# Fused attention, rational MLP and soft MoE on one core: combine in packed f32 tiles, first turn of g at its step's end, fourth w_in block in one piece, single x buffers, ten early pieces

## The chip, the cores and the metric

The kernel runs on one core of a Trainium2 chip. The metric is the device time of one execution in microseconds (us); lower is better. TensorE (PE, with its weight loads PEld), VectorE (DVE) and ScalarE (ACT) run their own instruction streams and meet at semaphores; SyncE (SP) issues nearly all DMAs.

## What is computed

```python
# attention: B=4, H=8, S=768, D=64; chunks of 32 queries, 16 keys to the left, 8 to the right, 8 memory keys
a = softmax(scale * q_c @ k_full.T); out[:, :, c] = a @ v_full
x = out.transpose(0, 2, 1, 3).reshape(3072, 512)
# rational MLP: w_in 512 x 2048, w_out 2048 x 512
h = x @ w_in
g = (a0 + a1*h + a2*h*h + a3*h*h*h) / (1 + |b0|*|h| + |b1|*h*h + 1e-6)
x = g @ w_out
# soft MoE: 8 experts, 4 slots each, w1 8 x 512 x 1024, w2 8 x 1024 x 512
logits = x @ phi
slot_input = softmax(logits, axis=0).T @ x
slot_out[e] = relu(slot_input[e] @ w1[e]) @ w2[e]
y = softmax(logits, axis=1) @ slot_out
```

## The kernel before

**Tokens.** 24 tiles of 128 tokens (4 batches of 6) go through a software pipeline. One step of each engine works on tile n (the hidden layer), the attention of tile n+1 (`nxt`), the transposes of g and the logits of n-1 (`prev`), the running column softmax of n-2 (`prev2`), and on TensorE the scores of n+2. g @ w_out is never formed per token: `Wp` = w_out @ phi is made once, and the slots accumulate g, which meets w_out at the end.

**Hidden layer.** `hidden` (lines 397 to 413) makes block f (512 columns) of h out of 12 matmuls of 512 columns, with x and w_in each split in a high and a low part (f32r). The blocks alternate between two PSUM banks `hb`. On ACT `hidden_reads` (710) copies hs, |h| and h squared out of the bank, and `inverse` and `inverse2` (721, 725) take Ln and Exp of the denominator; on DVE `cubic` (925) makes the numerator and the denominator q, and `activation` (940) makes g.

**Order within a TensorE step (476 to 548), written out by hand.** hidden 0; g_transposes 0 of prev; hidden 1; g_transposes 1, add_quadrants, p_transposes; hidden 2; attend (L386) of nxt; g_transposes 2 of prev; d_transpose of prev2; the first half of hidden 3; x_transposes of nxt; g_transposes 3; the second half of hidden 3; slots of prev2 (L456); logits of prev (L433); scores of n+2 (L362). `g_transposes` (four transposes, L339) all use the bank `gb`, so each waits until ACT has copied the one before (`gT_copy`, 729). `slots` waits for `dk_sb`, which `d_copy` (958) on DVE sets.

**DVE's order in a step (977 to 1020).** activation 3 of prev, softmax_max of nxt (with a memset for the first and the last tile of a batch, 897 to 902), cubic 0, activation 0, running_max, cubic 1, o_norm of nxt (908, it waits for attend), cubic 2, d_copy of prev2, x_low of nxt (919), activation 1, cubic 3, activation 2, accumulate. **ACT's order (767 to 828):** inverse 3 of prev, part_copy, hidden_reads 0, gT_copy 0, softmax_exp, inverse 0, hidden_reads 1, gT_copy 1, pT_copy (697), dispatch_exp, hidden_reads 2, gT_copy 2, inverse 1, x_high (703), gT_copy 3, hidden_reads 3, inverse 2. x_hi and x_lo have two buffers each.

**Expert weights.** w1 and w2 (32 MB) are 64 pieces of 512 KB ("quarters"), four to a stage, stages 0 to 7 for w1 and 8 to 15 for w2. Seven go to SBUF of their own and are loaded in steps 2 to 5 (285 to 290). The others (297 to 321) go to places that come free only with the last tile: three of the attention (waits on sc_psum, o_psum, xT_psum), sixteen of w_in (each four wait for one hidden block of the last tile, 307), then those of x, g, the temporaries and w_out, then places of used stages. SP issues all of it in order, and the stores of the result behind it (323 to 330).

**End.** The experts run as col-packed matmuls (32 slots wide, L599 and L637). `combine_turns` (613) transposes the softmax over slots, split in a high and a low part, with 48 matmuls of 64 x 128. `slot_rows` (641) replicates the experts' output for half the columns; ACT copies its upper 64 partitions and DVE makes the high and low parts of the other 64 in two steps (1113 to 1116). `combine` (647) then makes 24 f32r matmuls of 256 columns over all 128 partitions (L661), two to a pair of tiles; DVE and ACT copy pairs out in turn (1117, 880), and SP stores two to four pairs at a time. combine(0) runs between stages 13 and 14, combine(1) behind stage 15.

Of the kernel before, what the change touches and what calls it, by code (L numbers as in the profile page):

```python
# [5 lines left out]
def build(nc, qT_d, kw_d, vw_d, w_in, w_out, w_outT, cst_d, w1, w2, out):  # L6
# [23 lines left out]
    with ExitStack() as ctx:  # L30
# [27 lines left out]
        ab = sb("ab", [P, 2, 512])  # L58
        h2 = sb("h2", [P, 2, 512])
        tt = sb("tt", [P, 2, 512])  # L60
        qq = sb("qq", [P, 2, 512])
        early = sb("early", [P, 7168])
# [16 lines left out]
        xn = sc  # L79
        w_raw = [x.rearrange("p (k n) -> p k n", n=512)  # L80
# [5 lines left out]
        c_hl = gT[:, 4:16, :].rearrange("p a (t h s) -> p (a t) h s", h=2, s=NS)  # L86
# [4 lines left out]
        s_hi = g[:, 1, 512:1024]  # L91
# [14 lines left out]
        EARLY, ATT, WF, LATE, LEFT_G, TMP = 7, 3, 16, 2, 2, 5  # L106
# [9 lines left out]
        spots += [in_wout + QB * i for i in range(4)]  # L116
# [3 lines left out]
        def place(stage, c):  # L120
# [5 lines left out]
                   nc.alloc_sbuf_tensor_at("o_b", [P, 4, 2 * HC], f32, offset=in_tmp + 2 * QB),  # L126
# [8 lines left out]
        cT4 = nc.alloc_sbuf_tensor_at("cT4", [P, N, P], f32r, offset=in_wout + 16 * QUARTER)  # L135
        s4 = nc.alloc_sbuf_tensor_at("s4", [P, DM], f32r, offset=in_wout + 16 * QUARTER + 4 * N * P)
# [9 lines left out]
        o_bank = [[at[:, 0, :], at[:, 1, :], gb[:, :]], [at[:, 2, :], sl[:, :], at[:, 0, :], at[:, 1, :], gb[:, :]]]  # L146
# [74 lines left out]
        s4_act = sem("s4_act")  # L221
        s4_dve = sem("s4_dve")
# [14 lines left out]
        def g_bank(n, f):  # L237

            return at[:, f, :] if isinstance(n, int) and n == N - 1 and f < FC - 1 else gb
# [9 lines left out]
        def _(sp):  # L249
# [47 lines left out]
            for i in range(EARLY, 60):  # L297
# [36 lines left out]
        def _(pe):  # L334
# [62 lines left out]
            def hidden(b, t, f, kds=range(KD)):  # L397
# [9 lines left out]
                for kd in kds:  # L407
                    xs = slice(kd * P, kd * P + P)
                    mm(o, x_hi[:, p, xs], w_hi[:, f, kd, :], start=kd == 0, stop=False)  # L409
                    mm(o, x_hi[:, p, xs], w_lo[:, f, kd, :], start=False, stop=False)  # L410
                    i = mm(o, x_lo[:, p, xs], w_hi[:, f, kd, :], start=False, stop=kd == KD - 1)  # L411
# [3 lines left out]
            def g_transposes(b, t, f):  # L415
                n = b * T + t
                pe.wait_ge(g_done, FC * n + f + 1)
                last = isinstance(n, int) and n == N - 1 and f < FC - 1
                if not last:
                    need(pe, gT_sb, FC * n + f - (FC - 1 if isinstance(n, int) and n == N - 1 else 0))  # L420
# [55 lines left out]
            def step(b, t):  # L476
# [22 lines left out]
                if prev:  # L499
                    g_transposes(*prev, 0)  # L500
# [46 lines left out]
                if nxt2:  # L547
                    scores(*nxt2)

# [53 lines left out]
            def expert_turns(grp):  # L603
                for half in range(2):
                    pe.wait_ge((relu_dve, relu_act)[half], grp + 1)
                    if grp:
                        pe.wait_ge((cT_act, cT_dve)[half], N // 8)
# [5 lines left out]
            def combine_turns():  # L613
                pe.wait_ge(comb_step, 8)
                for j in range(N // 4):
                    if j < 2:
                        pe.wait_ge((hT_act, hT_dve)[j], 1)
                    else:
                        pe.wait_ge((cT_act, cT_dve)[j % 2], j // 2)
                    for m in range(4):  # L620
                        x = c_hl[:, 4 * j + m, :, :].rearrange("p a b -> p (a b)")
                        for r in (slice(0, 2 * NS), slice(2 * NS, 4 * NS)):
                            i = mm((gb, mb)[j % 2][r, m * P:m * P + P], x, ident[:, :], start=True, stop=True)
                    i.then_inc(cT_psum, 1)
# [22 lines left out]
            def combine(ch):  # L647
                cs = slice(HC * ch, HC * ch + HC)
                pe.wait_ge(s4_act, ch + 1)
                pe.wait_ge(s4_dve, 2 * ch + 2)  # L650
                if ch == 0:
                    pe.wait_ge(hT_act, 2)
                for j in range(PAIRS):
                    q = PAIRS * ch + (j - len(o_bank[ch]) if j >= len(o_bank[ch]) else -1)
                    if q >= 1:
                        pe.wait_ge((o_dve, o_act)[q % 2], q // 2 + 1)
                        pe.wait_ge((o_act, o_dve)[q % 2], (q + 1) // 2)
                    elif q == 0:
                        pe.wait_ge(o_dve, 1)
                    for m in range(2):  # L660
                        i = mm(o_bank[ch][j % len(o_bank[ch])][:, HC * m:HC * m + HC], cT4[:, 2 * j + m, :], s4[:, cs],  # L661
# [516 lines left out]
```

## Time and profile before

| | us |
|---|---|
| median of 3 runs | 527.86 (527.72 to 528.7) |
| profiled execution, its own time | 529.32 |
| its span | 527.4 |
| PE busy | 509.8 (97%) |
| DVE busy | 445.0 (84%) |
| ACT busy | 401.3 (76%) |

The span is what the profile shows of the execution. Busy time is the union of an engine's instructions. Stretches and rows below are in us from the span's start. In a timeline row the second number is the duration; successive instructions of an engine overlap in part, so prices are best read from start to start.

### The profile page before, as it was taken

The numbers are of one execution on the slowest core, as the hardware profiler recorded it, in microseconds if no ns is written. First come the engines' busy times: TensorE is split into PE (matmuls) and PEld (weight loads), VectorE is DVE, ScalarE is ACT, GpSimd is POOL, SyncE is SP. The second block draws the span as 40 slices with busy tenths as digits, with TensorE's granted clock in tenths as the row PEclk, the third lists the DMA queues.
The fourth block names the chain that finished last, engine by engine and source line by source line (L and its number), as shares of the span: only waits on it lengthen the run. The fifth ranks groups of instructions, "written<-read, shape, count | busy, mean of one in ns | idle before, by whom it ended". The sixth has DMA issues, their size and how long they took to land.

```text
span 527.4 us, 15890 instructions
## 1 busy us (share of the span) xinstructions
PE 509.8 (97%) x6610; PEld 387.0 (73%) x6610; DVE 445.0 (84%) x828; ACT 401.3 (76%) x778; POOL 0.2 (0%) x4
## 2 busy tenths in 40 slices
PE   8899999999999999999999999999999999999983
PEld 7667877877787778778777877787787777645543
DVE  5898999999999999999999999999999999642143
ACT  1878989888988898898889888988988898512032
POOL 0000000000000000000000000000000000000000
PEclk9999999999999999999999999999999999999996
DMA  8983275335122311312131322113122227999997
GB/s 346 416 334 119 64 262 180 121 105 181 43 93 70 103 43 62 101 57 87 62 103 43 88 74 78 68 62 102 58 87 61 83 81 289 412 408 409 408 410 298
DMA packets 23400, 85.31 MB, mean 162 GB/s; under 512 B 2593, under 2 KB 2721, under 8 KB 21409
## 3 DMA queue, kind: packets, MB, share of 16 engines
q1 hardware_dynamic: 23184, 84.09, 43.6%
q8 instruction: 53, 0.87, 0.7%
q10 hardware_dynamic: 144, 0.20, 0.1%
q14 instruction: 19, 0.15, 0.1%
HBM read 77.99 MB, written 6.29 MB: 160 GB/s over the span
## 4 chain that ended last, share of the span: by engine, by line
PE 89%; DMA 4%; ACT 2%; SPq 1%; DVE 1%; issue 1%; ACTq 0%
PE hb L409 18%; PE hb L411 17%; PE hb L410 17%; PE gb L339 9%; PE sl L456 4%; PE at L339 4%; PE mb L433 4%; PE at L386 3%; PE at L362 3%; DMA place<-w 2%; DMA g<-w_in 2%; PE at L599 1%; PE hb L599 1%; PE mb L441 1%; PE hb L345 1%; ACT w_hi L835 1%
## 5 line engine op out<-in xcount | busy, mean ns | idle before, releaser
L409 PE MATMUL hb<-w_hi,x_hi 128*128 128x512 f32 x384 | 162.6, 423 | 1.1 <-DVE x_lo L922 1.1
L411 PE MATMUL hb<-w_hi,x_lo 128*128 128x512 f32 x384 | 151.9, 396 | 0.0
L410 PE MATMUL hb<-w_lo,x_hi 128*128 128x512 f32 x384 | 151.3, 394 | 0.0
L716 ACT ACTIVATE hs<-hb 128x512 f32<-128x512 f32 x96 | 57.2, 596 | 48.0 <-PE hb L411 46.8
L411 PEld LDWEIGHTS hb<-w_hi,x_lo 128*128 128x128 f32 x384 | 72.2, 188 | 17.8
L409 PEld LDWEIGHTS hb<-w_hi,x_hi 128*128 128x128 f32 x384 | 72.2, 188 | 15.4 <-issue 1.4
L410 PEld LDWEIGHTS hb<-w_lo,x_hi 128*128 128x128 f32 x384 | 72.5, 189 | 11.9
L931 DVE SCALAR_TENSOR_TENSOR qq<-h,few,ab 128x512 f32<-128x512 f32 x96 | 71.9, 749 | 10.6 <-ACT h L718 10.4
L936 DVE SCALAR_TENSOR_TENSOR tt<-tt,cst,hs 128x512 f32<-128x512 f32 x96 | 72.2, 752 | 3.4
L723 ACT ACTIVATE qq<-qq,few 128x512 f32<-128x512 f32 x96 | 70.2, 732 | 5.8 <-DVE qq L931 4.4
L946 DVE SCALAR_TENSOR_TENSOR g<-tt,cst,qq 128x512 f32<-128x512 f32 x96 | 71.5, 747 | 2.3 <-ACT qq L727 0.2
L717 ACT ACTIVATE ab<-hb,cst 128x512 f32<-128x512 f32 x96 | 65.8, 686 | 0.0
L934 DVE TENSOR_TENSOR tt<-tt,hs 128x512 f32<-128x512 f32 x96 | 65.8, 686 | 0.0
L727 ACT ACTIVATE qq<-qq 128x512 f32<-128x512 f32 x96 | 60.7, 632 | 3.1
L339 PE MATMUL gb<-cst,g 128*128 128x128 f32 x380 | 58.5, 277 | 1.2 <-DVE g L1095 0.8
L718 ACT ACTIVATE h<-hb 128x512 f32<-128x512 f32 x96 | 57.9, 604 | 0.0
L733 ACT ACTIVATE gT<-gb 128x512 f32<-128x512 f32 x93 | 56.6, 609 | 0.7 <-PE gb L339 0.7
L929 DVE TENSOR_SCALAR tt<-hs,cst 128x512 f32<-128x512 f32 x96 | 52.1, 543 | 2.9 <-ACT hs L716 0.4
L339 PEld LDWEIGHTS gb<-cst,g 128*128 128x128 f32 x380 | 44.3, 140 | 13.4 <-DVE g L1095 2.6
L339 PE MATMUL at<-cst,sc 128*128 128x128 f32 x192 | 29.7, 277 | 1.5 <-ACT sc L694 1.1
L433 PEld LDWEIGHTS mb<-gT,Wp 128*32 128x32 f32 x736 | 20.9, 110 | 13.5 <-issue 13.5
L339 PEld LDWEIGHTS at<-cst,sc 128*128 128x128 f32 x192 | 23.7, 149 | 6.3 <-ACT sc L694 1.8
(154 smaller groups left out, 548.1 us busy)
## 6 DMA issues: line engine op xcount, KB each, us to landing
place<-w SPq DMA_DIRECT2D x60, 512.0 KB, 10.3
v_in<-v_windows SPq DMA_DIRECT2D x24, 520.0 KB, 3.8
kw<-k_windows SPq DMA_DIRECT2D x24, 512.0 KB, 4.6
qT<-q_t SPq DMA_DIRECT2D x24, 256.0 KB, 2.7
wout<-w_out_t SPq DMA_DIRECT2D x4, 1024.0 KB, 14.7
wout<-w_out SPq DMA_DIRECT2D x4, 1024.0 KB, 6.7
g<-w_in SPq DMA_DIRECT2D x3, 1024.0 KB, 10.5
out_dram<-o_c SPq DMA_DIRECT2D x6, 512.0 KB, 4.9
```

Of the source, the lines that this page charges most:

```text
L339: return mm(dst, src, ident[0:rows, 0:rows], start=True, stop=True, is_transpose=True)
L409: mm(o, x_hi[:, p, xs], w_hi[:, f, kd, :], start=kd == 0, stop=False)
L410: mm(o, x_hi[:, p, xs], w_lo[:, f, kd, :], start=False, stop=False)
L411: i = mm(o, x_lo[:, p, xs], w_hi[:, f, kd, :], start=False, stop=kd == KD - 1)
L717: A(ab[:, e, :], hb[:, e, :], ACT.Abs, scale=bc[:, 0:1])
L718: A(h2[:, e, :], hb[:, e, :], ACT.Square).then_inc(h_read, 1)
L723: A(qq[:, e, :], qq[:, e, :], ACT.Ln, bias=cq[:, 0:1]).then_inc(ln_done, 1)
L727: A(qq[:, e, :], qq[:, e, :], ACT.Exp, scale=-1.0).then_inc(r_done, 1)
L931: V.scalar_tensor_tensor(out=qq[:, e, :], in0=h2[:, e, :], scalar=bm[:, 1:2], in1=ab[:, e, :], op0=ALU.mult, op1=ALU.add).then_inc(q_done, 1)
L934: V.tensor_tensor(tt[:, e, :], tt[:, e, :], hs[:, e, :], ALU.mult).then_inc(poly_step, 1)
L936: V.scalar_tensor_tensor(out=tt[:, e, :], in0=tt[:, e, :], scalar=pc[:, 1:2], in1=hs[:, e, :], op0=ALU.add, op1=ALU.mult).then_inc(poly_st ...
L946: V.scalar_tensor_tensor(out=g[:, t % 3, 512 * f:512 * f + 512], in0=tt[:, e, :], scalar=pc[:, 0:1], in1=qq[:, e, :], op0=ALU.add, op1=ALU ...
```

## The change

It lays out memory anew (pT shares sc, one x_hi and one x_lo, one ab, no qq: q is written over h2), which makes room for ten early pieces in place of seven. On TensorE g_transposes 0 moves to the end of its own step, g_transposes 3 goes right behind 2, with 2 in the bank at[:, 2], attend moves behind d_transpose, hidden 3 is one piece, and x_transposes comes behind it. The combine is made of plain f32 matmuls over 32 rows, four to a round in different banks, with six transposes in place of the 48 matmuls.

```diff
-        pT = sb("pT", [P, HP * P])
-        x_hi = sb("x_hi", [P, 2, KD * P], f32r)
-        x_lo = sb("x_lo", [P, 2, KD * P], f32r)
+        x_hi = sb("x_hi", [P, KD * P], f32r)
+        x_lo = sb("x_lo", [P, KD * P], f32r)
-        early = sb("early", [P, 7168])
+        early = sb("early", [P, 10240])
+        pT = sc[:, :, :, :].rearrange("p a b c -> p (a b c)")
-        EARLY, ATT, WF, LATE, LEFT_G, TMP = 7, 3, 16, 2, 2, 5
+        EARLY, ATT, WF, LATE, LEFT_G, TMP = 10, 3, 16, 1, 2, 3
-        spots += [in_wout + QB * i for i in range(4)]
+        spots += [in_wout + QB * i for i in (0, 1, 2, 3, 6, 7)]
-        o_bank = [[at[:, 0, :], at[:, 1, :], gb[:, :]], [at[:, 2, :], sl[:, :], at[:, 0, :], at[:, 1, :], gb[:, :]]]
+        o_bank = [at[:, 0, :], at[:, 1, :], gb[:, :], at[:, 2, :], sl[:, :]]
...
         def g_bank(n, f):
+            if n == N - 1:
+                return at[:, f, :] if f < FC - 1 else gb
+            return at[:, 2, :] if f == 2 else gb
...
-                if n < 6:
+                if n < 7:
                     for i in range(2 * (n - 2), min(2 * n - 2, EARLY)):
...
-                elif i == RING - 4 or i == RING - 2:
-                    sp.wait_ge(si_psum, (i - RING + 4) // 2 + 1)
+                elif RING - 6 <= i < RING and (RING - i) % 2 == 0:
+                    sp.wait_ge(si_psum, (1, 2, 4)[(i - RING + 6) // 2])
...
@@ x_transposes
                 pe.wait_ge(soft, SOFT * n + SOFT)
+                need(pe, gT_sb, FC * (n - 2) + FC - 1)
...
@@ g_transposes
+                if n < N - 1 and f != 2:
+                    need(pe, gT_sb, FC * n + min(f, 2))
+                elif n < N - 1:
+                    need(pe, pT_sb, min(n + 3, N))
+                elif f == FC - 1:
+                    pe.wait_ge(gT_sb, FC * n)
...
@@ TensorE step
-                if prev:
-                    g_transposes(*prev, 0)
                 if here:
                     hidden(*here, 1)
...
                 if here:
                     hidden(*here, 2)
-                if nxt:
-                    attend(*nxt)
                 if prev:
                     g_transposes(*prev, 2)
+                if prev and not drain:
+                    g_transposes(*prev, 3)
...
                 if prev2:
                     d_transpose(*prev2)
                     spin_drain(b, t, 1)
-                if here:
-                    hidden(*here, 3, range(0, KD // 2))
+                if nxt:
+                    attend(*nxt)
+                if here:
+                    hidden(*here, 3)
...
                 if nxt:
                     x_transposes(*nxt)
-                if prev and not drain:
-                    g_transposes(*prev, 3)
-                if here:
-                    hidden(*here, 3, range(KD // 2, KD))
...
                 if nxt2:
                     scores(*nxt2)
+                if here:
+                    g_transposes(*here, 0)
...
@@ combine_turns
-                pe.wait_ge(comb_step, 8)
-                for j in range(N // 4):
...
+                pe.wait_ge(comb_step, 7)
+                pe.wait_ge(hT_act, 1)
+                for m in range(4):
+                    i = transpose(gb[:, m * P:m * P + P], c_all[:, m * P:m * P + P])
+                i.then_inc(cT_psum, 1)
+                pe.wait_ge(hT_dve, 1)
+                for m in range(2):
+                    i = transpose(mb[:, m * P:m * P + P], c_all[:, (4 + m) * P:(5 + m) * P])
+                i.then_inc(cT_psum, 1)
...
@@ combine
+                nb = len(o_bank)
+                for a in range(PAIRS // 4):
                     for m in range(2):
-                        i = mm(o_bank[ch][j % len(o_bank[ch])][:, HC * m:HC * m + HC], cT4[:, 2 * j + m, :], s4[:, cs],
-                               start=True, stop=True)
-                    i.then_inc(o_psums, 1)
+                        for r in range(4):
+                            j = 4 * a + r
+                            q = PAIRS * ch + (j - nb if j >= nb else -1)
+                            if m == 0 and q >= 0:
+                                pe.wait_ge((o_dve, o_act)[q % 2], q // 2 + 1)
+                            if m == 0 and q >= 1:
+                                pe.wait_ge((o_act, o_dve)[q % 2], (q + 1) // 2)
+                            rows = slice(NS * r, NS * r + NS)
+                            i = mm(o_bank[j % nb][:, HC * m:HC * m + HC], cT[rows, 2 * a + m, :], s_rows[rows, cs],
+                                   start=True, stop=True)
+                            if m == 1:
+                                i.then_inc(o_psums, 1)
...
@@ ACT
-                need(act, h_psum, FC * (n - 1))
-                A(x_hi[:, p, :], at[:, 2, :], ACT.Copy).then_inc(x_hi_done, 1)
+                need(act, h_psum, FC * n)
+                A(x_hi[:, :], at[:, 2, :], ACT.Copy).then_inc(x_hi_done, 1)
...
@@ hidden_reads
-                need(act, q_done, m - 1)
                 A(hs[:, e, :], hb[:, e, :], ACT.Copy).then_inc(h_copied, 1)
-                A(ab[:, e, :], hb[:, e, :], ACT.Abs, scale=bc[:, 0:1])
+                need(act, q_done, m)
+                A(ab[:, :], hb[:, e, :], ACT.Abs, scale=bc[:, 0:1])
+                need(act, g_done, m - 1)
                 A(h2[:, e, :], hb[:, e, :], ACT.Square).then_inc(h_read, 1)
...
@@ ACT step
+                if prev and not drain and n != 2:
+                    gT_copy(*prev, 0)
                 if here:
                     hidden_reads(*here, 0)
...
                     gT_copy(*prev, 2)
+                    gT_copy(*prev, 3)
                 if here:
                     inverse(FC * n + 1, 1)
                     inverse2(FC * n + 1, 1)
                 if nxt:
                     x_high(*nxt)
-                if prev and not drain:
-                    gT_copy(*prev, 3)
...
@@ ACT, end
-                A(s4[0:64, cs], mb[0:64, cs], ACT.Copy).then_inc(s4_act, 1)
+                A(s_rows[:, cs], mb[:, cs], ACT.Copy).then_inc(s_kept, 1)
...
@@ DVE step
+                if here:
+                    activation(*here, 1)
                 if nxt:
                     x_low(*nxt)
                 if here:
-                    activation(*here, 1)
                     cubic(*here, 3)
...
@@ DVE, end
-                dve.wait_ge(rep_psum, ch + 1)
-                V.tensor_copy(s_hi[64:128, cs].bitcast(f32r), mb[64:128, cs]).then_inc(s4_dve, 1)
-                dve.wait_ge(s4_dve, 2 * ch + 1)
-                V.tensor_tensor(s4[64:128, cs], mb[64:128, cs], s_hi[64:128, cs], ALU.subtract).then_inc(s4_dve, 1)
```

## Rows read from the trace of the kernel before

**Rows 1.** The page: busy time and share of TensorE.

```profile
PE 509.8 (97%) x6610; PEld 387.0 (73%) x6610; DVE 445.0 (84%) x828; ACT 401.3 (76%) x778; POOL 0.2 (0%) x4
```

**Rows 2.** Chain that ended last, 440 to 528: start, duration, what.

```profile
499.60 11.54 DMA place<-w
...
511.18 1.11 PE hb L637 x16
```

**Rows 3.** Windows: length, busy of PE, PEld, DVE, ACT, POOL; PEclk, DMA share, GB/s.

```profile
434.00:436.00 2.00, 2.00 (x16) 1.56 (x9) 1.89 (x3) 1.94 (x5) 0.00 (x0) 1.00 0.00 0
...
437.20:439.00 1.80, 1.80 (x11) 1.52 (x10) 1.66 (x4) 1.77 (x4) 0.00 (x0) 1.00 0.40 105
439.00:470.00 31.00, 29.33 (x258) 19.64 (x260) 22.76 (x47) 18.43 (x40) 0.00 (x0) 1.00 1.02 404
...
516.00:518.00 2.00, 2.00 (x11) 2.00 (x10) 1.68 (x3) 1.37 (x3) 0.00 (x0) 0.50 0.78 301
```

**Rows 4.** Timeline of TensorE, 214 to 252: start, duration, engine, line, operation.

```profile
232.65 1.06 PE L456 MATMUL sl<-g,dk 128*32 128x512 f32 x8
...
235.31 0.50 PE L409 MATMUL hb<-w_hi,x_hi 128*128 128x512 f32 x1
...
238.22 0.60 PE L339 MATMUL gb<-cst,g 128*128 128x128 f32 x4
...
245.63 0.86 PE L386 MATMUL at<-v_in,pT 64*32 64x65 f32 x64
246.42 0.66 PE L339 MATMUL gb<-cst,g 128*128 128x128 f32 x4
246.91 0.27 PE L339 MATMUL mb<-cst,dT 128*128 128x128 f32 x1
...
248.43 0.60 PE L339 MATMUL at<-cst,sc 128*128 128x128 f32 x4
248.87 0.60 PE L339 MATMUL gb<-cst,g 128*128 128x128 f32 x4
...
250.80 1.07 PE L456 MATMUL sl<-g,dk 128*32 128x512 f32 x8
```

**Rows 5.** Timeline of VectorE, 213 to 252.

```profile
216.31 0.75 DVE L931 SCALAR_TENSOR_TENSOR qq<-h,few,ab 128x512 f32<-128x512 f32 x1 [0.41 <-ACT h L718]
...
222.64 0.75 DVE L931 SCALAR_TENSOR_TENSOR qq<-h,few,ab 128x512 f32<-128x512 f32 x1
...
234.46 0.75 DVE L931 SCALAR_TENSOR_TENSOR qq<-h,few,ab 128x512 f32<-128x512 f32 x1 [0.36 <-ACT h L718]
...
240.41 0.75 DVE L931 SCALAR_TENSOR_TENSOR qq<-h,few,ab 128x512 f32<-128x512 f32 x1
...
246.53 0.17 DVE L912 TENSOR_SCALAR mx<-at 128x8 f32<-128x8 f32 x1 [0.22 <-PE at L386]
...
250.08 0.18 DVE L961 COPY dk<-mb 128x32 f32<-128x32 f32 x1
```

**Rows 6.** Timeline of ScalarE, 213 to 252.

```profile
232.76 0.60 ACT L716 ACTIVATE hs<-hb 128x512 f32<-128x512 f32 x1 [0.60 <-PE hb L411]
...
244.49 0.62 ACT L701 ACTIVATE pT<-at 128x512 f32<-128x512 f32 x1
...
249.07 0.60 ACT L707 ACTIVATE x_hi<-at 128x512 fp32r<-128x512 f32 x1
```

**Rows 7.** Timeline of all engines, 460 to 528.

```profile
480.60 1.09 PE L623 MATMUL gb<-cst,gT 128*64 128x128 f32 x16
...
486.34 3.64 PE L599 MATMUL at<-place,g 128*32 128x512 f32 x32
...
503.08 0.73 PE L661 MATMUL at<-s,cT 128*128 128x256 f32 x4
...
514.05 0.43 DVE L1116 TENSOR_TENSOR s<-mb,g 64x256 fp32r<-64x256 f32 x1
...
514.58 0.47 PE L661 MATMUL at<-s,cT 128*128 128x256 f32 x2 [1.03 <-ACT s L879]
```

More of the change, by code:

```diff
@@ L125, in build @@
         o_place = [nc.alloc_sbuf_tensor_at("o_a", [P, 8, 2 * HC], f32, offset=in_wout),
-                   nc.alloc_sbuf_tensor_at("o_b", [P, 4, 2 * HC], f32, offset=in_tmp + 2 * QB),
+                   nc.alloc_sbuf_tensor_at("o_b", [P, 4, 2 * HC], f32, offset=in_tmp + QB),
                    nc.alloc_sbuf_tensor_at("o_c", [P, 12, 2 * HC], f32, offset=in_early)]
@@ L132, in o_out @@
             return o_place[0][:, j, :] if j < 8 else o_place[1][:, j - 8, :]
-        cT4 = nc.alloc_sbuf_tensor_at("cT4", [P, N, P], f32r, offset=in_wout + 16 * QUARTER)
-        s4 = nc.alloc_sbuf_tensor_at("s4", [P, DM], f32r, offset=in_wout + 16 * QUARTER + 4 * N * P)
+        cT = nc.alloc_sbuf_tensor_at("cT", [P, N // 4, P], f32, offset=in_wout + 4 * QB)
+        s_rows = nc.alloc_sbuf_tensor_at("s_rows", [P, DM], f32, offset=in_wout + 4 * QB + N * P)
+        assert N * P + 4 * DM <= 2 * QB
         hb = ps("hb", [P, 2, 512])
@@ L408, in hidden @@
                     xs = slice(kd * P, kd * P + P)
-                    mm(o, x_hi[:, p, xs], w_hi[:, f, kd, :], start=kd == 0, stop=False)
-                    mm(o, x_hi[:, p, xs], w_lo[:, f, kd, :], start=False, stop=False)
-                    i = mm(o, x_lo[:, p, xs], w_hi[:, f, kd, :], start=False, stop=kd == KD - 1)
+                    mm(o, x_hi[:, xs], w_hi[:, f, kd, :], start=kd == 0, stop=False)
+                    mm(o, x_hi[:, xs], w_lo[:, f, kd, :], start=False, stop=False)
+                    i = mm(o, x_lo[:, xs], w_hi[:, f, kd, :], start=False, stop=kd == KD - 1)
                 if kds[-1] == KD - 1:
@@ L606, in expert_turns @@
                     if grp:
-                        pe.wait_ge((cT_act, cT_dve)[half], N // 8)
+                        pe.wait_ge((cT_act, cT_dve)[half], 1)
                     for j in range(4):
@@ L613, in combine_turns @@
             def combine_turns():
-                pe.wait_ge(comb_step, 8)
-                for j in range(N // 4):
[L616 to L624, printed above, removed]
+                pe.wait_ge(comb_step, 7)
[7 more added lines that the diff above has]
+                i.then_inc(cT_psum, 1)
             def expert_out(stage):
@@ L700, in pT_copy @@
                 need(act, o_psum, n)
-                A(pT[:, :], at[:, 2, :], ACT.Copy).then_inc(pT_sb, 1)
+                A(pT, at[:, 2, :], ACT.Copy).then_inc(pT_sb, 1)
             def x_high(b, t):
@@ L793, in step @@
                     part_copy(*prev2)
-                if prev:
+                if n == 2:
+                    gT_copy(*prev, 0)
+                if drain:
                     gT_copy(*prev, 0)
@@ L869, in _ @@
                 if grp:
-                    act.wait_ge(cT_psum, N // 4)
+                    act.wait_ge(cT_psum, 2)
                 A(hT[grp][:, 0:4, :].rearrange("p a b -> p (a b)"), gb[:, :], ACT.Copy).then_inc(hT_act, 1)
-                for j in range(0, N // 4, 2) if grp == 0 else ():
-                    act.wait_ge(cT_psum, j + 1)
+                if grp == 0:
+                    act.wait_ge(cT_psum, 1)
                     act.wait_ge(si_psum, FC)
-                    A(cT4[:, 4 * j:4 * j + 4, :].rearrange("p a b -> p (a b)"), gb[:, :], ACT.Copy).then_inc(cT_act, 1)
+                    A(cT[:, 0:4, :].rearrange("p a b -> p (a b)"), gb[:, :], ACT.Copy).then_inc(cT_act, 1)
             for ch in range(2):
@@ L882, in _ @@
                     act.wait_ge(o_psums, q + 1)
-                    A(o_out(ch, j), o_bank[ch][j % len(o_bank[ch])], ACT.Copy).then_inc(o_act, 1)
+                    A(o_out(ch, j), o_bank[j % len(o_bank)], ACT.Copy).then_inc(o_act, 1)
         @block.vector
@@ L921, in x_low @@
                 dve.wait_ge(x_hi_done, n + 1)
-                V.tensor_tensor(x_lo[:, p, :], at[:, 2, :], x_hi[:, p, :].bitcast(f32), ALU.subtract).then_inc(x_lo_done, 1)
+                V.tensor_tensor(x_lo[:, :], at[:, 2, :], x_hi[:, :].bitcast(f32), ALU.subtract).then_inc(x_lo_done, 1)
             def cubic(b, t, f):
@@ L930, in cubic @@
                 dve.wait_ge(h_read, m + 1)
-                V.scalar_tensor_tensor(out=qq[:, e, :], in0=h2[:, e, :], scalar=bm[:, 1:2], in1=ab[:, e, :],
+                V.scalar_tensor_tensor(out=h2[:, e, :], in0=h2[:, e, :], scalar=bm[:, 1:2], in1=ab[:, :],
                                        op0=ALU.mult, op1=ALU.add).then_inc(q_done, 1)
@@ L1083, in _ @@
             dve.wait_ge(comb_step, 5)
-            V.tensor_tensor(Lall[:, :, :], Lall[:, :, :], cb(cr), ALU.mult).then_inc(comb_step, 1)
-            dve.wait_ge(comb_step, 6)
-            V.tensor_copy(c_hl[:, :, 0, :].bitcast(f32r), Lall[:, :, :]).then_inc(comb_step, 1)
-            dve.wait_ge(comb_step, 7)
-            V.tensor_tensor(c_hl[:, :, 1, :].bitcast(f32r), Lall[:, :, :], c_hl[:, :, 0, :], ALU.subtract
-                            ).then_inc(comb_step, 1)
+            tiles = Lall[:, :, :].rearrange("p (a r m) s -> p m a r s", r=4, m=2)
+            order = c_all.rearrange("p (a m r s) -> p m a r s", m=2, r=4, s=NS)
+            scale = cr.rearrange("p (a r m) -> p m a r", r=4, m=2)
+            for m in range(2):
+                V.tensor_tensor(order[:, m], tiles[:, m], scale[:, m].unsqueeze(3).broadcast_to([P, N // 8, 4, NS]), ALU.mult
+                                ).then_inc(comb_step, 1)
             for grp in range(2):
@@ L1097, in _ @@
                 if grp:
-                    dve.wait_ge(cT_psum, N // 4)
+                    dve.wait_ge(cT_psum, 2)
                 V.tensor_copy(hT[grp][:, 4:8, :].rearrange("p a b -> p (a b)"), mb[:, :]).then_inc(hT_dve, 1)
                 if grp == 0:
+                    dve.wait_ge(cT_psum, 2)
                     dve.wait_ge(si_psum, FC)
-                    for j in range(1, N // 4, 2):
-                        dve.wait_ge(cT_psum, j + 1)
-                        V.tensor_copy(cT4[:, 4 * j:4 * j + 4, :].rearrange("p a b -> p (a b)"), mb[:, :]).then_inc(cT_dve, 1)
+                    V.tensor_copy(cT[:, 4:6, :].rearrange("p a b -> p (a b)"), mb[:, 0:2 * P]).then_inc(cT_dve, 1)
             for ch in range(2):
```

33 lines of the change are left out of this document (10 added, 23 removed).

## The prediction

> **What bounds the kernel now.** First the page's busy line: TensorE is busy 97% of the span [rows 1], so ask where it is the clock of the work and where it only looks so. The chain that ended last, read backwards, answers for the end: its longest link is a load of weights from 499.60 to 511.14, and TensorE's last expert matmuls start at 511.18, when it lands [rows 2]. The windows say when that stream begins: between 434 and 436 the DMA queues move nothing, from 437.2 they start, and from 439 they run at 404 GB/s with a share of 1.02 [rows 3]. That is the end of the last tile's first hidden block, whose w_in places the loads may then take. So the span has two parts: up to that moment (437.0) TensorE's steps set the time, behind it the volume of weights does. A piece of 512 KB (0.524 MB) takes 1.30 us at 404 GB/s; 54 of 64 pieces are behind that point, 70 us of the 74 that pass until 511.14, the rest being the start and the stores that already mix in.
>
> In the first part one step is 18.15 us (slots to slots, 232.65 to 250.80), and I find no wait of TensorE inside it [rows 4]. DVE has waits of its own there [rows 5], so it has a little slack. What matters for a reordering is how close each handover is: d_copy starts at 250.08 and ends at 250.26, slots needs it at 250.80 [rows 4, 5], 0.5 of slack; pT is copied by 245.11, attend starts at 245.63 [rows 4, 6], another 0.5.
>
> **Part 1, three more early pieces.** They are loaded in steps 5 and 6, when the queues are mostly empty; I cost them at nothing. Behind 437 there are 51 pieces in place of 54: 3 x 1.30 = 3.9 us less. The places of w_out now wait for si_psum up to 4, and the queue has three pieces fewer as a cushion; about three pieces (4 us) remain at that wait, so no hole. Bounds: 0 (the earlier stores of the first half mix in ahead of the last load, and TensorE has 5 us more of lead to make them early) and 4.5. I take 3.9, since the stores stand behind all loads in SP's order. The Trainium skill ("DMA: Bandwidth & Descriptors", Queues, rings and completion order) says that descriptors of one queue are consumed in ring order; by that the whole 3.9 stands, and nothing here shows it directly.
>
> **Part 2, order of the step.** The work of TensorE is the same: four hidden blocks, four turns of g at 0.44 (248.43 to 248.87) and so on [rows 4]. Entering or leaving the small tiles costs about 0.1 (scores to hidden: the block takes 2.91 from 235.31 to 238.22, against 2.80 for twelve matmuls in a row); there are as many such changes as before, give or take one. I take 0, bounds -0.2 and +0.1 a step. The Trainium skill ("TensorEngine Tiling (Array Packing)", Key Properties) says that a change of tiling mode drains the engine; charged at that 0.1 for each change of mode, one change more or less in 21 steps would make 2 us, which is inside these bounds.
>
> The handovers are another matter. **d_copy to slots:** DVE does o_norm, cubic 2, d_copy behind attend. From the start of attend it is 0.90 to o_norm and 3.55 on to d_copy (246.53 to 250.08), 0.18 for it and 0.05 to TensorE: 4.68 [rows 4, 5]. Before, slots came 5.17 behind attend. Now attend has gone behind the turns 2 and 3 of g and d_transpose, and between it and slots stand only itself (0.79), hidden 3 (2.91) and x_transposes (0.44): 4.14 [rows 4]. TensorE waits 0.54 in each step. Everything from slots on is then late: slots, logits, scores 2.66 (232.65 to 235.31), less about 0.1 for the exit; turn 0 of g 0.44; hidden 0 to the end of hidden 2 10.32 less 0.44 for that turn (235.31 to 245.63); turns 2 and 3 and d_transpose 0.99 [rows 4]. 4.68 + 2.56 + 0.44 + 9.88 + 0.99 = 18.55, a closed loop from attend to attend. With a restart behind the wait (some 0.05) a step is 18.6, +0.45.
>
> **pT_copy to turn 2 of g:** turn 2 now writes the bank at[:, 2] and waits for pT_copy, 1 us ahead of where attend did. pT's time follows from the end of hidden 3: x_transposes to x_hi 0.64 (248.43 to 249.07), x_hi about 0.5 to the next start, hs to q of block 3 1.70 (232.76 to 234.46), q 3 to q 0 of the next tile 5.95 with DVE at work throughout (234.46 to 240.41), then 4.70 until pT is there (244.49 + 0.62): 13.5 [rows 4 to 6]. From attend this is 3.70 + 13.5 = 17.2, and TensorE comes at 4.68 + 2.56 + 0.44 + 9.88 = 17.56. No wait in an ordinary step. Where the next tile opens or closes a batch the memset makes it 6.33 in place of 5.95 (216.31 to 222.64) [rows 5]: 17.6 with the wake-up, so +0.6 for the step in place of +0.45. So it is a second fence right behind the first.
>
> The 20 loops from step 2 to 22 hold 7 such tiles: 13 x 0.45 + 7 x 0.6 = 10.0. Step 1 has no slots, but the pT loop is 18.4 there: +0.6. Turn 0 of g for tile 22 now stands ahead of the last tile's first block: +0.4. **The stream of weights begins 11.0 late.**
>
> Costed at nothing: the single x buffers (activation 1 and x_low come behind d_copy, two operations of about 0.7, so x_lo is ready 5.9 behind attend; hidden 0 of the next tile starts 4.68 + 2.56 + 0.44 = 7.7 behind it; with the slots wait gone 1.2 of cover is left); single ab and h2 in place of qq (their waits name DVE results at least 2 us old); pT in sc. On ACT gT_copy 0 moves into an idle gap before hidden_reads 0, and x_high ahead of hidden_reads 3 delays that by 0.9, which is in the loop above.
>
> **Part 3, the end.** 48 matmuls from 480.60 to 486.34 [rows 7] become six transposes, 0.7: TensorE is 5.0 earlier, but behind it the last load decides, so this is worth nothing now. Of `slot_rows` DVE's second step goes: ACT's copy of 0.4 alone, -0.5 of the 0.96 behind it. The new combine has 24 plain f32 matmuls of 32 rows; no row shows that form. From the col-packed ones (32 instructions of 512 columns, four abreast, in 3.64 us) one f32 matmul of 256 columns is 2 x 0.228 = 0.455 [rows 7]. Four abreast the 24 take 6 x 0.455 = 2.7; one by one 10.9; now the first combine takes 4.8 and the second 5.2, by the copies. L386, 64 rows by 32 columns, 65 wide, issues 64 in 0.79, less than four abreast would allow (64 x 65 x 2 columns at 2.4 GHz, over 4, is 0.87), so row tiles do overlap; I take four abreast. Then the first pair comes 0.5 later than now, or over 1 us at half clock, which the granted clock of 0.50 at 516 (1.2 of 2.4 GHz, behind waits) makes likely [rows 3]; but behind it the stores, 3.1 MB at 0.4 MB/us, are 8 us and hide most. Sum of the end: -0.5 + 0.6 = 0, bounds -1 and +6 (one by one). The Trainium skill ("TensorEngine Tiling (Array Packing)", Theoretical Speedup) gives up to four times for 32-row tiles; by that the 2.7 stands, which no row here shows.
>
> **Sum.** +11.0 - 3.9 + 0 = +7.1. The profiled execution would go from 529.3 (span 527.4, 1.9 around it) to 536.4. It was 1.5 above the median of the runs shown, 527.9, to which I apply the same difference: 535.0.
>
> **Rivals.** (a) **The handovers hide, the shorter stream wins: faster.** The place is slots: if DVE reaches d_copy 0.5 earlier than I read, or TensorE loses only what its fewer changes of mode give back, the loops cost 0 to 1. Then 0.4 + 0.5 - 3.9 = -3.0: 524.9. It decides where the loss per loop stays under (3.9 - 1.0) / 20 = 0.14 us. Against it: 4.68 against 4.14 is read start to start in one step. Chance 0.10. (b) **Only the pT fence holds**, at 18.39 a step and 18.75 with a memset (slots free): 13 x 0.24 + 7 x 0.6 + 1.0 - 3.9 = +4.4: 532.3. Chance 0.15. (c) **The gain of the stream is lost** to stores or to a half clock behind a longer idle: +11: 538.9. Chance 0.12. (d) **The row tiles don't overlap:** combine(1) 10.9 in place of 5.2, and more at half clock: +6 to +12: 541 to 547. Chance 0.05. (e) Gain and loss cancel within 0.2%: 0.05. My forecast, 533.5 to 537: 0.53.
>
> **How the numbers follow.** 535.0 is the likeliest. The range leaves out about half of (a), and (d): 529.5 to 538.5 (its low end reaches a loss of half the loops; its high end most of (c)). About 0.2% (1.06 us) is what a measurement of this kernel can tell from no change. Slower: 0.53 + 0.15 + 0.12 + 0.05 = 0.85; same 0.05; faster 0.10.
>
> **What would show it.** Steps of 18.6 from slots to slots, and of about 18.75 in seven; a wait of TensorE at L456 for DVE's dk of some 0.5, 20 times; its wait at the turn 2 for ACT's pT only in the tiles with a memset; the first load of the dense stream at 448; the last landing near 518; 70 us between the two. Wrong: steps of 18.15, or the wait at another line; a last load that lands as late behind the first block as before (74); L661's successors one behind another at 0.45.

## The result, and the profile after

The changed kernel takes 535.29 us (median of 4 runs, 534.73 to 536.95) against 527.93 us (4 runs): ratio 1.0138, 95% interval 1.012 to 1.0156, slower by 7.4 us. Its profiled execution was the longest of the four, 536.95 us with a span of 535.2.

The step first. The issue of q for a later tile follows the scores at once, so SP's timeline dates the steps (start, duration, what):

```profile
203.53 0.33 SPq L262 DMA_DIRECT2D qT<-q_t  x1
...
222.27 0.33 SPq L262 DMA_DIRECT2D qT<-q_t  x1
...
241.06 0.33 SPq L262 DMA_DIRECT2D qT<-q_t  x1
...
259.65 0.33 SPq L262 DMA_DIRECT2D qT<-q_t  x1
```

Steps of 18.74, 18.79 (both with a memset) and 18.59 us stand where all steps were 18.15 [rows 4]. The waits name what closes them (engine, line, waited for: total, times, longest):

```profile
PEld sl L460 <- DVE dk L970: 14.6, 23, 0.7
...
PE sl L460 <- DVE dk L970: 9.0, 23, 0.4
```

slots (L456 before, L460 now) waits for DVE's dk 23 times. No such wait stood in the repeated steps before. The matmul itself waits 0.4, its weight load 0.7: the row of PEld counts from the end of the last load, which ran ahead of the matmuls, so the time lost is the matmul's own, 9.0 us in all. TensorE's timeline after, in the step that answers to [rows 4]:

```profile
233.60 0.86 PE L386 MATMUL at<-v_in,sc 64*32 64x65 f32 x64
...
237.30 0.60 PE L339 MATMUL at<-cst,sc 128*128 128x128 f32 x4
...
238.30 1.06 PE L460 MATMUL sl<-g,dk 128*32 128x512 f32 x8 [0.40 <-DVE dk L970]
...
240.96 0.66 PE L339 MATMUL gb<-cst,g 128*128 128x128 f32 x4
...
251.13 0.60 PE L339 MATMUL at<-cst,g 128*128 128x128 f32 x4
...
252.21 0.86 PE L386 MATMUL at<-v_in,sc 64*32 64x65 f32 x64
```

and DVE's, which answers to [rows 5]:

```profile
234.50 0.17 DVE L921 TENSOR_SCALAR mx<-at 128x8 f32<-128x8 f32 x1 [0.95 <-PE at L386]
...
238.06 0.18 DVE L970 COPY dk<-mb 128x32 f32<-128x32 f32 x1
```

attend at 233.60, o_norm 0.90 later, dk copied at 238.24, slots at 238.30: 4.70 behind attend. x_transposes start at 237.30; where nothing waits (attend_pt below, 250.12 to 250.64) slots follow them by 0.52, which would have been 237.82. So 0.48 is lost. Both attends are 18.61 apart.

Now the end. The last tile's first hidden block ends at 448.64 in place of 437.19 (437.0 in the prediction is the start of the turn behind it), 11.4 later. Its last matmul in TensorE's timeline, before and after:

```profile
436.80 0.39 PE L411 MATMUL hb<-w_hi,x_lo 128*128 128x512 f32 x1
...
448.24 0.40 PE L412 MATMUL hb<-w_hi,x_lo 128*128 128x512 f32 x1
```

The chain that ended last, from there on:

```profile
492.48 15.13 DMA place<-w
507.61 0.04 issue
507.65 1.93 PE hb L637 x32
...
516.18 5.84 PE hb L637 x64
```

This is not the end of [rows 2]. The load on the chain is that of stage 13, not the last one; behind it come stage 13, combine(0) (509.58 to 516.18) and stages 14 and 15 in 5.84 us without a wait for weights. 5.84 us for 64 matmuls is the half clock (3.63 in attend_pt_hold and old_combine, at full clock), as the windows show (stretch, length, busy of PE, PEld, DVE, ACT, POOL; PEclk, DMA share, GB/s):

```profile
513.00:514.00 1.00, 0.64 (x5) 0.42 (x4) 1.00 (x2) 0.90 (x2) 0.00 (x0) 0.89 1.07 391
514.00:515.00 1.00, 1.00 (x12) 0.89 (x9) 0.06 (x1) 0.00 (x0) 0.00 (x0) 0.50 1.05 383
...
518.00:520.00 2.00, 2.00 (x28) 0.85 (x23) 0.00 (x0) 0.00 (x0) 0.00 (x0) 0.50 0.97 401
...
521.00:522.00 1.00, 0.97 (x20) 0.29 (x12) 0.00 (x0) 0.00 (x0) 0.00 (x0) 1.00 1.02 418
```

From 514 until the clock comes back between 520 and 521 TensorE runs at 1.2 in place of 2.4 GHz. The other three executions have spans of 532.9 to 533.5 at a mean clock of 0.997 against 0.990 here, 1.7 to 2.3 us shorter. The place where it is lost can be seen: with TensorE late, the queues have no stores to move, and the DMA share falls to 0.51, 0.22, 0.00 and 0.55 in the four us from 523 to 527, while in attend_pt below it stays at 0.79 or more in each us from 506 to 519.

### The profile page after: what moved, and what is told of

Read it like the earlier page. It is cut to its first block, busy times and chain, and to the rows that moved or that the text cites. A ratio compares the mean times of both kernels' runs of the same rounds, so it can differ in the third digit from the quotient of the medians.

```text
span 535.2 us, 15816 instructions
## 1 busy us (share of the span) xinstructions
PE 510.9 (95%) x6568; PEld 386.4 (72%) x6568; DVE 439.5 (82%) x821; ACT 399.0 (75%) x776; POOL 0.2 (0%) x4
## 4 chain that ended last, share of the span: by engine, by line
PE 74%; DVE 11%; issue 6%; DMA 5%; ACT 2%; SPq 1%; DVEq 0%; ACTq 0%
PE hb L410 13%; PE hb L412 13%; PE hb L411 13%; PE gb L339 7%; PE sl L460 5%; PE at L339 4%; PE mb L437 4%; PE at L386 3%; PE at L362 3%; DMA place<-w 3%; DVE h L940 3%; DVE tt L943 3%; DVE tt L938 2%; DMA g<-w_in 2%; PE hb L637 1%
## 5 line engine op out<-in xcount | busy, mean ns | idle before, releaser
L410 PE MATMUL hb<-w_hi,x_hi 128*128 128x512 f32 x384 | 158.6, 413 | 1.7 <-DVE x_lo L931 1.6
L412 PEld LDWEIGHTS hb<-w_hi,x_lo 128*128 128x128 f32 x384 | 72.1, 188 | 17.6
L729 ACT ACTIVATE h<-h,few 128x512 f32<-128x512 f32 x96 | 70.6, 736 | 9.0 <-DVE h L940 9.0
L940 DVE SCALAR_TENSOR_TENSOR h<-h,few,ab 128x512 f32<-128x512 f32 x96 | 71.9, 749 | 5.2 <-ACT h L724 4.9
L955 DVE SCALAR_TENSOR_TENSOR g<-tt,cst,h 128x512 f32<-128x512 f32 x96 | 71.5, 746 | 2.3 <-ACT h L733 0.2
L733 ACT ACTIVATE h<-h 128x512 f32<-128x512 f32 x96 | 60.7, 632 | 3.0
L339 PE MATMUL gb<-cst,g 128*128 128x128 f32 x288 | 44.7, 278 | 0.8 <-DVE g L1105 0.8
L739 ACT ACTIVATE gT<-gb 128x512 f32<-128x512 f32 x70 | 42.9, 613 | 0.7 <-PE gb L339 0.7
L339 PEld LDWEIGHTS gb<-cst,g 128*128 128x128 f32 x288 | 33.1, 140 | 8.6 <-DVE g L1105 2.6
L712 ACT ACTIVATE x_hi<-at 128x512 fp32r<-128x512 f32 x24 | 14.3, 597 | 29.9 <-PE at L339 29.9
L460 PE MATMUL sl<-g,dk 128*32 128x512 f32 x192 | 25.6, 605 | 9.0 <-DVE dk L970 9.0
## 6 DMA issues: line engine op xcount, KB each, us to landing
wout<-w_out_t SPq DMA_DIRECT2D x4, 1024.0 KB, 15.2
```

The costliest lines, as they stand in the source:

```text
L339: return mm(dst, src, ident[0:rows, 0:rows], start=True, stop=True, is_transpose=True)
L410: mm(o, x_hi[:, xs], w_hi[:, f, kd, :], start=kd == 0, stop=False)
L412: i = mm(o, x_lo[:, xs], w_hi[:, f, kd, :], start=False, stop=kd == KD - 1)
L729: A(h2[:, e, :], h2[:, e, :], ACT.Ln, bias=cq[:, 0:1]).then_inc(ln_done, 1)
L733: A(h2[:, e, :], h2[:, e, :], ACT.Exp, scale=-1.0).then_inc(r_done, 1)
L940: V.scalar_tensor_tensor(out=h2[:, e, :], in0=h2[:, e, :], scalar=bm[:, 1:2], in1=ab[:, :], op0=ALU.mult, op1=ALU.add).then_inc(q_done, 1)
```

## The experiments

Theory A is the prediction's: attend moved too close to slots, the handover of dk (DVE) closes a loop of 18.6 us, the copy of pT (ACT) is a second fence right behind it, the late stream of weights then costs what the steps lost, less three pieces. Rival B lays the long steps on the single buffers or on changes of tiling mode. Rivals C and D concern the end. The kernel before ran beside each group, with medians of 528.39 and 528.31 us.

**Attend back behind hidden 2 (attend_back).**

```diff
@@ TensorE step, of the changed kernel
                 if here:
                     hidden(*here, 2)
+                if nxt:
+                    attend(*nxt)
...
-                if nxt:
-                    attend(*nxt)
                 if here:
                     hidden(*here, 3)
```

> The changed kernel with attend put back right behind hidden 2, all else as changed. Theory A (the handover d_copy to slots closes the loop, with the pT fence right behind it): between attend and slots stand 0.79 + 0.99 + 2.9 + 0.44 = 5.1 us, more than the 4.68 of DVE, so the wait at slots goes; attend now waits for pT instead, the loop through pT is 13.5 + 0.1 + 0.79 + 0.99 + 2.8 = 18.2 to 18.4 in ordinary steps and 0.35 more with a memset. 4 to 6 us faster than the changed kernel, 530 to 532 us. Rival B (the steps are long because of the single x buffers or of changes of tiling mode): steps stay at 18.6, 535 us.

Measured: 527.46 us (10 runs), ratio to before 0.999 (0.9975 to 1.0005), 7.8 us below the changed kernel. Steps are 18.19, with a memset 18.51 and 18.57. Rival B falls: single buffers and all else are still there. The wait went to the pT fence: attend starts 0.09 to 0.10 behind the end of pT's copy in each of the four steps between 190 and 250. The profile books what is left of the wait as issue, not on ScalarE, so this rests on the distance. ScalarE's copy and TensorE's attend, in a step with a memset:

```profile
210.22 0.62 ACT L706 ACTIVATE sc<-at 128x512 f32<-128x512 f32 x1
...
210.93 0.85 PE L386 MATMUL at<-v_in,sc 64*32 64x65 f32 x64 [0.36 <-issue]
```

18.19 is the low end of the 18.2 to 18.4 expected, and the last tile's first block ends 7.5 earlier (441.11), so the gain is larger than the 4 to 6 us expected.

**Scores ahead of slots (scores_first).**

```diff
@@ TensorE step, of the changed kernel
+                if nxt2:
+                    scores(*nxt2)
                 if prev2:
                     slots(*prev2)
...
-                if nxt2:
-                    scores(*nxt2)
                 if here:
                     g_transposes(*here, 0)
```

> The changed kernel with the scores of the tile after next ahead of slots, all else as changed. Theory A: 0.8 us more work stands between attend and slots (4.9 in place of 4.1), so TensorE no longer waits for dk; the fence of pT at the turn 2 of g is now what sets the step: 18.39 in ordinary steps, 18.75 with a memset, about 2.5 us faster than the changed kernel, 532 to 533 us. If pT is no fence (only slots matters): steps of 18.1, 9 us faster, 526 us. Rival B (x buffers, tiling modes): no change, 535 us.

Measured: 532.36 us (4 runs, 532.24 to 532.84), ratio 1.0075 (1.006 to 1.009). This leaves attend where the change put it and only fills the gap. SP's timeline:

```profile
219.09 0.33 SPq L262 DMA_DIRECT2D qT<-q_t  x1
...
237.88 0.33 SPq L262 DMA_DIRECT2D qT<-q_t  x1
...
256.29 0.33 SPq L262 DMA_DIRECT2D qT<-q_t  x1
```

18.79 with a memset (18.72 in the step before it), 18.41 without; the forecast was 18.75 and 18.39. TensorE's timeline shows the second fence in place of the first, in the step with the memset:

```profile
231.66 0.63 PE L339 MATMUL at<-cst,g 128*128 128x128 f32 x4 [0.47 <-ACT sc L706]
```

L706 is pT_copy. In ordinary steps no idle time is marked, but turn 2 starts 0.14 behind the end of that copy there too (268.35 to 268.49). The dk wait at slots is gone from the repeated steps. So the two fences stand behind one another, and taking the first away gives back 0.2 a step where 0.45 were lost.

**And pT_copy ahead of gT_copy 1 (scores_pt_first).**

```diff
@@ ScalarE step, on top of scores_first
                     hidden_reads(*here, 1)
+                if nxt:
+                    pT_copy(*nxt)
                 if prev:
                     gT_copy(*prev, 1)
-                if nxt:
-                    pT_copy(*nxt)
```

> As the one with scores ahead of slots, and on ScalarE pT_copy ahead of gT_copy 1. Theory A: pT is there 0.48 earlier, the loop through it is 17.9 (18.3 with a memset), below TensorE's own 18.05 to 18.15, so both fences are gone: the steps are 18.1 as before the change, the dense stream of weights starts 0 to 1 us behind where it started before the change, and the three early pieces pay: 523 to 526 us, faster than both kernels. Rival B: 535 us. Rival C (the end has become longer by itself, not by the late stream): steps of 18.15 but a time of 527 or more.

Measured: 526.17 us (10 runs, 525.39 to 528.31), ratio 0.9964 (0.9951 to 0.9977): faster than both. One copy swapped on ScalarE gives 6.2 us. Ordinary steps are 18.13, but those with a memset 18.33 and 18.38: a remainder that the forecast of 18.1 for all steps did not have. 18.75 less the 0.48 of the swap is 18.27, which the expectation gives as 18.3 and yet calls below 18.15. The fence is still there in those steps: turn 2 starts 0.15 behind the end of pT's copy (210.08 to 210.23), in ordinary ones 0.38 (191.63 to 192.01).

**Three pieces late (three_late).**

```diff
@@ SP, of the changed kernel
-                if n < 7:
-                    for i in range(2 * (n - 2), min(2 * n - 2, EARLY)):
+                if n < 6:
+                    for i in range(2 * (n - 2), min(2 * n - 2, EARLY - 3)):
...
                     if (k - ATT) % 4 == 0:
                         sp.wait_ge(h_psum, (N - 1) * FC + (k - ATT) // 4 + 1)
+                    if k == ATT:
+                        for late in range(EARLY - 3, EARLY):
+                            load_quarter(late // 4, late % 4)
```

> The changed kernel with only seven pieces early; the other three are loaded when the first block of the last tile is done, at the head of the dense stream, into their own places. Theory A: the stream is 3 x 1.3 us longer and the end follows it: +3.9 us, 539 us; from the first block of the last tile to the end 90.5 in place of 86.6. Rival (the end no longer hangs on the stream but on TensorE's clock and the copies): 0 to +1.5 us.

Measured: 540.01 us (4 runs, 538.74 to 540.66), ratio 1.0215 (1.0195 to 1.0235), 4.7 us above the changed kernel. The chain that ended last:

```profile
510.96 10.85 DMA place<-w
...
521.85 1.11 PE hb L640 x16
```

Here the last load is on the chain, 73.4 us behind the last tile's first block (448.4). With the three pieces early it lands 69.0 behind that block in scores_first (446.3 to 515.3). So three pieces are 4.4 us of stream, 1.5 each, and the time follows with 4.7: the expected 3.9 was too little.

**The new order alone, on the kernel before (order_alone).** TensorE's, ScalarE's and VectorE's step lists with `g_bank`, `g_transposes` and `x_transposes` of the changed kernel; memory, seven pieces, double x and the old combine as before.

```diff
@@ on the kernel before (TensorE's part)
                     hidden(*here, 2)
-                if nxt:
-                    attend(*nxt)
                 if prev:
                     g_transposes(*prev, 2)
+                if prev and not drain:
+                    g_transposes(*prev, 3)
...
+                if nxt:
+                    attend(*nxt)
+                if here:
+                    hidden(*here, 3)
...
+                if here:
+                    g_transposes(*here, 0)
```

> The kernel before with the new order of the steps alone (TensorE, ScalarE and VectorE lists, banks and waits of the turns of g), and its own memory, seven early pieces, two x buffers and old combine. Theory A: steps of 18.6 and 18.75 as in the changed kernel, the dense stream begins 11 us late, nothing is given back behind it: 538.5 to 539.5 us, about +2.1%. Rival B (single x buffers, single ab, q over h2 make the steps long): steps of 18.15, 528 us.

Measured: 539.31 us (4 runs, 538.97 to 539.82), ratio 1.0214 (1.0198 to 1.0229): +11.0 us, with double buffers. Steps of 18.60, and 18.73 to 18.78 with a memset. Its waits:

```profile
PEld sl L462 <- DVE dk L968: 14.6, 23, 0.7
...
PE sl L462 <- DVE dk L968: 9.0, 23, 0.4
```

The same totals as in the changed kernel to the tenth. The order alone makes the long steps, without a single x buffer or a changed place in memory.

**Both fences gone (attend_pt).** attend_back with the swapped copy of scores_pt_first.

```diff
@@ both, on the changed kernel
                     hidden(*here, 2)
+                if nxt:
+                    attend(*nxt)
...
-                if nxt:
-                    attend(*nxt)
...
                     hidden_reads(*here, 1)
+                if nxt:
+                    pT_copy(*nxt)
                 if prev:
                     gT_copy(*prev, 1)
-                if nxt:
-                    pT_copy(*nxt)
```

> The changed kernel with attend right behind hidden 2 and pT_copy ahead of gT_copy 1. Theory A: neither dk nor pT is a fence now (pT 0.48 earlier takes 18.19 and 18.55 below TensorE's own 18.1), so all steps are 18.1; the first block of the last tile ends at 437 to 438, and 84 (clock held) to 86.6 us (clock halved in the experts) later the span ends: 523 to 526 us, faster than both kernels by 0.4 to 0.9%. Rival (a third fence follows, for instance the memset's on DVE): memset steps stay above 18.3, 526 us.

Measured: 523.52 us (4 runs, 522.98 to 523.82), ratio 0.9916 (0.9899 to 0.9932): 4.8 us faster than before and 11.8 faster than the changed kernel, the fastest version of the study. SP's timeline:

```profile
199.01 0.33 SPq L262 DMA_DIRECT2D qT<-q_t  x1
...
217.17 0.33 SPq L262 DMA_DIRECT2D qT<-q_t  x1
...
235.31 0.33 SPq L262 DMA_DIRECT2D qT<-q_t  x1
...
253.40 0.33 SPq L262 DMA_DIRECT2D qT<-q_t  x1
```

18.16, 18.14, 18.09. In ordinary steps TensorE's own work sets the time, 0.06 below the old 18.15. With a memset dk still just touches: the weight load of slots waits for it, and slots start 0.60 behind x_transposes in place of 0.52.

```profile
214.41 0.16 PEld L460 LDWEIGHTS sl<-g,dk 128*32 128x32 f32 x8 [0.24 <-DVE dk L970]
```

The last tile's first block ends at 437.05, 0.14 ahead of before. The chain's end:

```profile
495.20 10.85 DMA place<-w
506.09 1.11 PE hb L637 x16
```

The last load lands 69.0 behind the block, where it took 74.0 before, and decides again.

**The old combine (old_combine).** attend_pt with the combine, its turns, banks and DVE's two steps of the kernel before, and four w_out places.

```diff
@@ on attend_pt
-                pe.wait_ge(s_kept, ch + 1)
+                pe.wait_ge(s4_act, ch + 1)
+                pe.wait_ge(s4_dve, 2 * ch + 2)
...
-                            i = mm(o_bank[j % nb][:, HC * m:HC * m + HC], cT[rows, 2 * a + m, :], s_rows[rows, cs],
+                        i = mm(o_bank[ch][j % len(o_bank[ch])][:, HC * m:HC * m + HC], cT4[:, 2 * j + m, :], s4[:, cs],
                                    start=True, stop=True)
```

> As attend_pt, with the old combine (48 matmuls as turns, 24 f32r matmuls of 128 rows, DVE's two steps), its banks and four w_out places in place of six. Theory A (the end hangs on the last load until stage 15 and then on the stores): from the first block of the last tile to the end 86.5 in place of 84.3, most of it DVE's second step and the 5 us of turns that make TensorE late for the first combine: +1.5 to +2.5 us against attend_pt. Rival C (the new combine is slower, its first pairs come later): 1 to 2 us faster than attend_pt. Rival D (all of the gain behind the last tile is the three pieces): the same within 0.5.

Measured: 526.04 us (6 runs, 525.77 to 527.35), ratio 0.9965 (0.9951 to 0.9978), 2.5 us slower than attend_pt. Its chain has no load in the end:

```profile
500.37 1.86 PE hb L640 x32
502.23 0.45 PE at L664 x2
...
507.03 3.63 PE hb L640 x64
...
511.22 0.71 PE mb L648 x2
```

Stages 14 and 15 run from 507.03 in one piece; the weights are there. TensorE is late because its 48 turns still take 5.7 us (479.68 to 485.42). So the new combine is worth 2.5 us here. The turns were not run apart from the matmuls, but the traces place the gain ahead of stage 15: its last matmul ends at 510.66 with the old combine and at 507.20 in attend_pt, while the rest of the span is no shorter with the new one (14.0 against 13.4). The new combine(0) is not shorter either, as shown further down; the turns are, by 5.0.

With only seven pieces early TensorE reached the last matmuls as their weights did [rows 2], with ten the weights are earlier and TensorE has to be as well. Four traces put this in a table, in us from the end of the last tile's first block to the end of the span:

| | seven pieces early | ten |
|---|---|---|
| old combine | 88.7 (order_alone) | 86.8 (old_combine) |
| new combine | 88.6 (three_late) | 84.2 (attend_pt) |

With seven pieces the new combine earns 0.1, with ten 2.6; the three pieces earn 1.9 behind the old combine and 4.4 behind the new. Each number is one execution, none of them at half clock in stages 14 and 15, and order_alone has the memory of the kernel before.

**Matmuls to hold the clock (attend_pt_hold).**

```diff
@@ TensorE, on attend_pt
             slot_rows(0)
+            spin(12, hb[:, 1, :], cst)
             expert_out(13)
```

> As attend_pt, with 12 matmuls without use (1.3 us) on TensorE ahead of stage 13, where it waits for weights. If the clock falls because of that wait, the granted clock stays at 1.0 in experts 14 and 15 in every run: the highest runs vanish (spread under 1 us) and the median is 0 to 1 us lower. If it falls because of the copies in combine(0), the spread stays as it is.

Measured: 525.99 us (8 runs, 525.84 to 529.62), ratio 0.9971 (0.9952 to 0.9989): 2.5 us slower than attend_pt, where 0 to 1 us faster was expected if the wait mattered, and the spread did not vanish (3.8 us in 8 runs, against 0.8 in 4 of attend_pt). The twelve matmuls take 2.7 us (495.20 to 497.97), not the 1.3 put down for them, and the wait that they fill was only 0.46 in attend_pt, so stage 13 starts 2.3 later (497.97 against 495.66), and the end follows. That is a second sign, beside old_combine, that TensorE's own time counts at this end once ten pieces are early. On the clock the run decides little: the wait ahead of stage 13 was longer in the changed kernel (0.86), and a run of 529.62 us at a mean clock of 0.988 is there with the wait filled. Why the clock falls in some executions and not in others stays open.

## Why the prediction was right, and where it was not

**Size and sign.** Forecast 535.0 in a range of 529.5 to 538.5, measured 535.29; for the profiled execution 536.4 forecast, 536.95 measured.

**d_copy to slots: right.** The forecast was 4.68 from attend to slots and a step of 18.6; measured 4.70 and 18.61. Order alone on the kernel before shows it without any other part.

**The pT fence: right, in its own loop and as second fence.** 18.39 and 18.75 were forecast for it alone, scores_first has 18.41 and 18.79. In the changed kernel itself the forecast was no wait in ordinary steps and one with a memset; 18.73 to 18.79 fits 18.75, and turn 2 starts 0.14 behind the end of pT's copy in those steps, as in scores_first, against 0.27 in ordinary ones. The written sums were looser than their results: 0.99 + 3.70 + 13.5 is 18.2, not 18.39, and 17.6 against 17.56 makes +0.5, not +0.6. What was missing is a restart of 0.14 behind the copy, and 0.1 more in front of x_transposes (4.79 from turn 2 in scores_first, for 0.99 + 3.70); 13.5 itself was measured as 13.48.

**The late stream: 11.0 forecast, 11.4 measured** (437.19 to 448.64). The two steps at the head account for most of the rest: by the issue behind its scores step 2 ends 0.95 later than before (72.09 to 73.04), where I had put 0.6 on step 1.

**What costs nothing: right.** With attend_pt all steps run at 18.08 to 18.17 with single x buffers, single ab and q over h2.

**Three pieces: the right term, sized too small.** 1.30 us a piece from the windows' rate gave 3.9; three_late against the others gives 4.4 between block and last landing and 4.7 in the time. Rival (c), that the gain is lost, falls. Behind the old combine it would in part have been: 1.9, by the table.

**The end: wrong in the step, right in the sum.** The prediction said that behind the turns "the last load decides" and that these 5.0 us are "worth nothing now". That holds with seven pieces early (0.1 by the table), but the change itself makes them ten: old_combine shows 2.5 us for the new combine as a whole, because the earlier load makes TensorE's lead count. And the new combine's own matmuls were taken as short. They do go four abreast, as taken: a matmul of this kind shows as two records (the twelve of attend_pt_hold as 24), and groups of four records start 0.21 apart, so a round of four matmuls takes 0.43 where 0.455 was taken, and rival (d) falls. But TensorE is not free after them. The timeline of the first combine after:

```profile
509.51 0.48 PE L665 MATMUL at<-s_rows,cT 32*128 32x256 f32 x2
...
509.85 0.37 PE L665 MATMUL gb<-s_rows,cT 32*128 32x256 f32 x1
...
510.06 0.37 PE L665 MATMUL gb<-s_rows,cT 32*128 32x256 f32 x1
...
510.28 0.37 PE L665 MATMUL gb<-s_rows,cT 32*128 32x256 f32 x1
...
510.68 0.69 DVE L1125 COPY o_a<-at 128x512 f32<-128x512 f32 x1 [5.69 <-PE at L665]
...
511.43 0.77 PE L665 MATMUL at<-s_rows,cT 32*128 32x256 f32 x4 [0.35 <-DVE o_a L1125]
...
513.52 0.56 PE L665 MATMUL sl<-s_rows,cT 32*128 32x256 f32 x1 [0.36 <-DVE o_a L1125]
```

A group of four pairs is ready only together, 1.2 us after its start, while the copies stand idle, and then TensorE waits for the copies: 5.6 us for combine(0) in attend_pt (497.5 to 503.2), 6.6 at a clock that fell during it, against 4.8 of the old one. Behind the last landing this does not show: the end follows it by 15.1 to 15.2 us in attend_pt, scores_first and three_late, with the new combine, and by 15.2 in order_alone, with the old. The stores cover it, as the prediction had it. Ahead of the last landing it can: in attend_back, at full clock, the chain runs through stage 13's load (499.73) and combine(0) to the last matmuls at 510.13. By the 69.0 of the others the last load lands at 510.1 there, so the two paths are level. The 16.3 in the profile before goes with its half clock in combine(1) [rows 3].

**What would show it.** The step, the line of the wait and the stream near 448 came as stated. The last landing near 518 did not set the end in the profiled execution; that was stage 13's load at 507.6 and the half clock behind it. The errors (0.4 too little in front, the pieces 0.5 to 0.8 too little, the clock not in the sum) nearly cancel; that the median came within 0.3 us of the forecast is partly luck, the steps' 18.6 is not.

The sum of the parts, now measured: the order +11.0 on the kernel before, the three pieces -4.7 by three_late, the new combine about nothing without them. That makes +6.3 against the measured +7.4; 0.4 to 0.5 of the gap is the kernel before itself, whose median was 527.93 in one group and 528.39 and 528.31 in the others, the rest stays open. Once the order costs nothing, pieces and combine together are worth 4.8 (attend_pt against the kernel before): 2.3 without the new combine (old_combine) and 2.5 for it.

## What to carry to other kernels

When an order on one engine is changed, work out for each handover the time from the producer's trigger to the consumer before and after; a busy engine that has never waited can sit 0.5 us from a closed loop that every iteration then pays. Fences stand behind one another, so removing one gives back only the distance to the next, and the remedy may be one copy's place on a third engine. And what a piece of work is worth depends on which queue decides the end: a faster combine earned nothing (0.1 us) until the weights were early too (2.6).

## What the runs showed of the hardware that was not expected

The clock of TensorE fell to half during a combine whose waits for copies are 0.35 us each. It did so in the profiled executions of the changed kernel (granted clock 0.50 from 514) and of scores_pt_first (from 506), where TensorE had waited 0.86 and 0.95 us for weights ahead of stage 13; in attend_back, scores_first and attend_pt that wait was 0.46 to 0.51, the waits for copies were the same, and the clock held through stage 15. In three_late it fell at 507, behind a wait of 2.15. That is an order of events in six executions, not a cause shown: the fall in the first two comes 6 us and more behind the long wait. With stages 14 and 15 behind it the half clock was 5.84 us in place of 3.63. The other executions of the changed kernel have a mean clock of 0.997 against 0.990, so a forecast of a tail like this has two values some 2 us apart.
